# One wait of TensorE moved: the last plain row sum is waited for in front of layer 2 of the first factored pass, not its layer 1

## The reference, cut to what matters

```python
N, D, E, F = (1536, 512, 4, 1024)
p = domain_probs / (domain_probs.sum(-1, keepdims=True) + 1e-09)
for e in range(E):
    h = np.maximum(x @ w1[e], 0.0)      # layer 1
    out += p[:, e:e + 1] * (h @ w2[e])  # layer 2 and the row sum
```

## Time and profile before

| | us |
|---|---|
| median of three timed runs | 738.40 |
| the profiled execution | 737.88 |
| its span (first to last instruction) | 736.1 |
| TensorE (PE) busy | 707.5 |
| VectorE busy | 427.6 |
| ScalarE busy | 291.6 |
| bytes moved / mean rate | 101.60 MB / 138 GB/s |

### The profile page before, as it was taken

One profiled execution on the slowest core, in us unless ns is written; L12 is line 12 of the kernel. 1 busy time (PEld: TensorE's weight loads), 2 busy tenths in 40 slices (PEclk: granted clock), 3 DMA queues, 4 the chain that ended last, 5 costly groups with the idle time before them and its releaser, 6 DMA issues.

```text
span 736.1 us, 12384 instructions
## 1 busy us (share of the span) xinstructions
PE 707.5 (96%) x4530; PEld 583.7 (79%) x4531; DVE 427.6 (58%) x1061; ACT 291.6 (40%) x651; POOL 68.1 (9%) x97
## 2 busy tenths in 40 slices
PE   5789999999989999999999999999999999999997
PEld 4578898888979889989988897898898985444444
DVE  4877674452976764782769469666542255544341
ACT  3655454351436614632624455056031202533430
POOL 2612000000000000000000000200100012332221
PEclk9999999999999999999999999999999999999999
DMA  9894732111523303213070723123224279599900
GB/s 200 215 219 94 145 68 63 42 37 62 225 76 124 115 1 116 74 41 115 1 285 9 280 84 115 24 91 115 86 86 172 87 287 356 204 396 396 386 8 21
DMA packets 88240, 101.60 MB, mean 138 GB/s; under 512 B 54617, under 2 KB 54893, under 8 KB 87281
## 3 DMA queue, kind: packets, MB, share of 16 engines
q1 hardware_dynamic: 85520, 96.14, 40.5%
q0 software_dynamic: 2656, 4.66, 2.0%
HBM read 88.32 MB, written 12.96 MB: 138 GB/s over the span
## 4 chain that ended last, share of the span: by engine, by line
PE 78%; DVE 12%; DMA 5%; issue 2%; SPq 1%; ACT 1%; POOL 0%; POOLq 0%; DVEq 0%; ACTq 0%
PE ps L1761 14%; PE ps L1763 14%; PE ps L1762 14%; PE ps L2023 6%; PE ps L2025 6%; PE ps L2024 6%; PE ps L2172 4%; PE ps L2144 4%; DMA sets<-in_moe_w 3%; DVE wb_lo L1341 2%; PE ps L1823 1%; PE ps L1795 1%; PE ps L1969 1%; PE ps L1809 1%; DVE xt_lo L1320 1%
## 5 line engine op out<-in xcount | busy, mean ns | idle before, releaser
L2023 PE MATMUL ps<-xt_hi,wb_hi 128*128 128x384 f32 x280 | 94.1, 336 | 4.8 <-DVE acc L1206 3.0
L2025 PE MATMUL ps<-xt_hi,wb_lo 128*128 128x384 f32 x280 | 93.6, 334 | 0.0
L2024 PE MATMUL ps<-xt_lo,wb_hi 128*128 128x384 f32 x280 | 93.6, 334 | 0.0
L954 ACT ACTIVATE h_raw<-ps 128x384 f32<-128x384 f32 x80 | 39.3, 491 | 90.8 <-PE ps L2025 88.9
L1762 PE MATMUL ps<-v_lo_acc,hb_hi 128*128 128x512 f32 x180 | 70.1, 390 | 0.0
L1761 PE MATMUL ps<-xt_hi,w_hi 128*128 128x384 f32 x184 | 64.2, 349 | 0.3 <-DVE h_lo L1197 0.3
L1355 DVE TENSOR_TENSOR h_raw<-ps,h_raw 128x384 f32<-128x384 f32 x80 | 41.4, 553 | 37.3 <-PE ps L2025 37.3
L1763 PE MATMUL ps<-xt_hi,w_lo 128*128 128x384 f32 x184 | 61.8, 336 | 0.0
L890 ACT ACTIVATE h_hi<-ps 128x384 fp32r<-128x384 f32 x48 | 23.6, 492 | 96.2 <-PE ps L1763 71.0
L1762 PE MATMUL ps<-xt_lo,w_hi 128*128 128x384 f32 x184 | 61.6, 335 | 0.0
L960 ACT ACTIVATE hb_hi<-h_raw 128x384 fp32r<-128x384 f32 x80 | 40.9, 526 | 45.3 <-DVE h_raw L1355 45.2
(11 more groups left out here) (268 smaller groups left out, 1402.9 us busy)
## 6 DMA issues: line engine op xcount, KB each, us to landing
sets<-in_moe_w SPq DMA_DIRECT2D x72, 512.0 KB, 5.0
w_raw<-in_moe_w SPq DMA_DIRECT2D x20, 512.0 KB, 5.3
acc<-in_moe_w SPq DMA_DIRECT2D x10, 768.0 KB, 5.3
stage<-in_moe_w SPq DMA_DIRECT2D x8, 512.0 KB, 4.5
stage<-in_k SPq DMA_DIRECT2D x16, 192.0 KB, 4.8
acc<-in_v SPq DMA_DIRECT2D x4, 768.0 KB, 6.8
x_rows<-acc SPq DMA_DIRECT2D x4, 768.0 KB, 6.7
out_rows<-acc SPq DMA_DIRECT2D x4, 768.0 KB, 8.3
```

Of the source, the lines that this page charges most:

```text
L954: nc.scalar.activation(h_raw[:, f, half * GT:(half + 1) * GT], ps[:, bank, 0:GT], ACT.Copy).then_inc(put_by, 1)
L2023: mm(to, wb_hi[w], hi(c), start=(c == 0 and not onto), stop=False, skip_group_check=onto)
L2024: mm(to, wb_hi[w], lo(c), start=False, stop=False, skip_group_check=onto)
L2025: last = mm(to, wb_lo[w], hi(c), start=False, stop=(c == HALF_D - 1), skip_group_check=onto)
```

## The change

The wait for `acc_ok` at 14 leaves the place in front of the first pass's layer 1 and goes to the head of that pass's `rows_out`, which is its layer 2. Nothing else differs: no instruction is added or removed, and the order on every engine is the same.

```diff
             def rows_out(t, fill):
 
                 b = PASSES[t][0]
+                if t == 0:
+                    pe.wait_ge(acc_ok, 2 + GR * G)
                 for tt in range(TPH):
                     m = TPH * t + tt
                     if m >= 2:
@@
             pe.wait_ge(o_lo, TASKS)
             pe.wait_ge(pt_ready, 2 * TASKS)
             pe.wait_ge(h_ok, 2 + FC * G)
-            pe.wait_ge(acc_ok, 2 + GR * G)
             for t in range(len(PASSES)):
                 factors(t, route_fill if t == SWITCH else lambda k: None)
```

## The result

| | before | changed |
|---|---|---|
| median of 20 timed runs, us | 739.41 | 736.96 |
| lowest and highest | 736.84, 742.14 | 735.80, 738.80 |
| profiled span | 736.1 | 735.0 |

The ratio is 0.9967, with a 95% interval of 0.9956 to 0.9979: 2.4 us faster, between 1.6 and 3.3. I had forecast 738.1 us, 0.3 us faster and at most 1.3. The measured 736.96 is inside the range, and the direction is the one forecast, but the gain is larger: it lies above the 0.3 to 1.3 us that had a chance of 0.80, and it is just over the 0.3% for which "faster" had a chance of 0.10.

What follows compares the result with a forecast made beforehand. TensorE's stream was taken to set the pace until about 260 us. A 3.26 us shift less stalls of 1.8 and 1.0 and restarts of 0.16 leaves 0.3: 738.4 - 0.3 = 738.1 us, range 736.0 to 739.8.

Steps and rivals of the forecast that it cites:

- The wait goes, 3.26 us of shift: TensorE, first pass: factored layer 1 starts at 213.26 without its wait, an undisturbed shift of 3.26 us.
- SyncE's chain stays, and the loads become the pace: SyncE still writes at 216.22 and issues loads at 222.00 and 222.43; ScalarE's splits wait for them, 3.3 us at the first.
- the first stall: TensorE, step 1 of layer 1: S3 waits for ScalarE's fourth put and starts at 228.6, 1.8 us lost.
- Landings of 4.5 and 7.2 us, so 0.3 us of gain: Layer 2's two weight loads land at 226.5 and 229.6, so only 0.3 us of the shift stays.
- The second stall: TensorE, step 2: S1 waits for VectorE's second join of step 1, behind the second load; 1.0 us lost.
- the other end: If the second load lands after 6.2 us, S1's stall goes and the gain is about 1.3 us.
- the slower rival: TensorE's clock falls to half for 3 us during the new stalls: 1.2 us slower, 739.6; chance 0.07.
- The sum: Whole kernel: profiled 737.88 minus 0.3 is 737.6; as a median, 738.4 minus 0.3 is 738.1 us.
- The starting point: Kernel before: median of three runs taken as 738.4 us, 0.5 us above the profiled execution.
- The new wait in front of layer 2 costs nothing: TensorE, layer 2: `acc_ok` is at 14 since 216.18 and layer 2 starts near 245.5, so no cost.
- The page's estimate: Layer 2's weight loads: 3.8 us each by the skill's fit, second landing at 226.2, gain about 2.1 us; the prediction rejected it.

Runs made afterwards that it cites:

- later splits: Changed kernel with the first pass's layer 2 weight splits one step later on ScalarE and VectorE: ratio to the kernel before 0.9931, again 0.9942.
- earlier loads: Changed kernel with SyncE's write of the `acc` tiles in two halves, each load behind its own half: ratio to the kernel before 0.9928.
- later loads: Changed kernel with SyncE writing the `acc` tiles twice before the loads are issued: ratio to the kernel before 1.0057.
- the kernel before with the second write: Kernel before with SyncE writing the `acc` tiles once more, to a spare tensor, before the loads: ratio 1.0061.

## Why the prediction was right or wrong

- *The wait goes, 3.26 us of shift.* Right: 3.23 us where nothing takes it back.
- *SyncE's chain stays, and the loads become the pace.* Right, and shown from both sides (later splits, earlier loads, later loads). ScalarE's idle time was forecast as 3.3 us and is 3.49; TensorE waits for the fourth put, forecast about 1.5 us, measured 1.71. That the first stall came out so well (1.8 us forecast, 1.88 measured against the undisturbed pace) is in part luck: in this profile and the next SyncE's write took 0.4 us longer than in the three of the kernel before (6.18 and 6.19 for 5.78 to 5.81), while TensorE started S3 only 0.05 us after the end of the put, where I had counted 0.26. In the third profile, without the longer write, the stall was 1.45.
- *Landings of 4.5 and 7.2 us, so 0.3 us of gain.* This term was mis-sized. In all three profiles of the changed kernel the two issues of line 538 took 0.92 us, as in the later passes, and the second load landed after 6.3, 6.2 and 6.0 us. The second stall that I expected, for the join, was forecast as 1.0 us and measured 0.16 us in the first profile and at most 0.02 in the other two. The stretch is shorter by 1.0, 1.1 and 1.6 us: 1.2 in the mean, near the 1.3 that I kept as the other end.
- *The clock.* Here I asked half the question. I put a price on a fall behind the *new*, shorter pauses and called it the slower rival. That the *old* pause might already cost such a fall in a part of the executions never entered the sum, because the one profile had 1.00 through it. The experiments say that it does: 1.47 us in the one profile where nothing else hides it. The new pause of 1.3 to 1.7 us showed no fall in three profiles.
- *The sum.* With 2 falls in 5 profiles the clock adds 0.6 us, together 1.8 us, inside the measured 1.6 to 3.3. The clocks of the timed runs say more. On the two chips of the experiments that timed both kernels, the mean granted clock averages 0.9936 and 0.9932 over 39 and 28 runs of the kernel before, and 0.9956 and 0.9953 over 10 and 12 runs of the changed one. The difference of 0.0020 is, as an estimate, 0.0020 x 736 = 1.5 us of work at the full clock, and with the 1.2 us of the stretch it gives 2.7, near the 2.4. It takes in lowered stretches elsewhere, but those ahead of the change, 20 to 44 us into the span, lie where both kernels run the same matmuls, and those in its last few us find TensorE done. An average of 1.5 us would be about one fall of 3 us in every execution, and three of the five profiles show none. How often the clock falls behind the pause, and for how long, remains open.
- *The starting point.* The median of the three runs shown was low, 738.40 against 739.41 for 20 runs. That is why the absolute forecast missed by only 1.1 us although the gain was off by 2.1. This was luck: two errors of opposite sign.
- *The new wait in front of layer 2 costs nothing.* Right: TensorE starts layer 2 at 244.84 without a pause. (In the kernel before it had started at 245.64; the 245.8 that I compared with was read too roughly.)
- *The page's estimate.* The fit in the Trainium skill (DMA: Bandwidth & Descriptors, the section on the anatomy of one DMA) gave an estimate of 3.8 us a load and 2.1 us of gain at this place. The rows stay against it: the first load landed 4.4 us after its issue, the second 6.0 to 6.3, and the gain here is 1.0 to 1.6.

The version with later splits and the version with earlier loads beat both kernels: 0.9931 and 0.9942 in two timings, and 0.9928.

## What to carry to other kernels

When a wait moves off one engine, look for who else waits for the same semaphore: here SyncE did, and already in the kernel before its loads landed just as ScalarE reached their splits. A split or copy that waits for a load should not stand in front of work that another engine needs soon; moving it by one step made the stretch 1.6 to 2.3 us shorter. Count a pause of TensorE at its length and at what its clock may cost behind it, and look at more than one profile before calling that nothing.

## What the runs showed of the hardware that was not expected

- Behind the same pause of 3.0 us TensorE's granted clock stayed at 1.00 in three profiles and fell to 0.50 for 3 us or a little more in two, 1.47 us in the undisturbed comparison. With the pause filled with transposes, neither of two profiles shows it.
- The second of two equal load issues on SyncE's queue was slow in the three profiles of the kernel before (1.37, 1.24 and 1.30 us for the pair) and not in the ten others that issue the pair (0.91 to 0.92), among them two of kernels with the same pause. What slows it is open.
- The same write of the `acc` tiles took 5.8 us (5.76 to 5.84) from its issue to that of the next DMA in ten places and 6.2 us in four, with both values among the profiles of the changed kernel, and once, in the kernel before with the second write, 7.3 us. Why is open; 0.4 us of it is 0.4 us of TensorE's pause in the changed kernel.
